# A four-stage fp32 chain on TensorE: three tile loads and one weight's sums moved in hand-written engine lists

## The chip, the cores and the metric

The kernel runs on one core of one Trainium2 chip. The metric is the device time of one execution in microseconds; the time before is the median of three.

## What is computed

Attention with a per-head decay (a retention layer) over 8 x 8 heads of 576 tokens and 64 dimensions, then two feed-forward blocks over the 4608 tokens:

```python
ret = scale * (q @ k.T) * Dmat          # Dmat = gamma ** (i - j) below the diagonal
x = (ret @ v) as [4608, 512]
h = max(max(x @ w1, x @ w2), x @ w3)    # w1..w3: 512 x 768
x = h @ w_out                           # 768 x 512
a, b = x @ u1, x @ u2                   # 512 x 1024
y = ((a * b) @ u3) @ u_out              # 1024 x 1024, 1024 x 512
```

The kernel multiplies u3 and u_out with each other first, beside the attention, so that the last two products are one of 1024 x 512.

## The kernel before, in words

After the attention four matrix stages follow, named B (the three products with w1 to w3 and their maximum), C (w_out), I (u1, u2 and their product) and O (u3 u_out). Each stage goes over six tiles of 768 tokens; a tile is read by 9, 2, 8 or 2 units (`PER_TILE`), each with a weight of its own. The units are numbered through: stage B has 0 to 53, C 54 to 65, I 66 to 113, O 114 to 125. Tiles are numbered through too (`tau`): 0 to 5, 6 to 11, 12 to 17, 18 to 23; so stage C's first tile is 6 and its third is 8, and weights 9 and 10 are stage C's, 11 to 18 stage I's, 19 and 20 stage O's.

A unit is a 2 x 2 block product done with seven products instead of eight (P1 to P7). So each tile is needed as seven blocks: four that are loaded (positions 0, 3, 6, 2, `load_raw`) and three sums of them, and a fourth sum that replaces position 3 (`combine`, four instructions on GpSimd that write positions 4, 1, 3, 5). Each weight is treated likewise: `load_weight` on SyncE (tiles `wraw` and `w21`), `sum_weight` (four instructions on GpSimd, counted by `w_summed`). fp32 accuracy comes from two rounded parts: ScalarE casts a block to its high part (`chi` for tokens, `whi` for weights), VectorE subtracts it from the block for the low part (`clo`, `wlo`), and TensorE multiplies high by high, high by low and low by high (lines 1261 to 1263).

The program has one loop over the iterations `it` = 0 to 126 on each engine, and within an iteration each engine's list is fixed; nothing is reordered at run time. TensorE does in iteration `it`: P1(it), P5(it-1), P4(it-1), P6(it), P3(it-1), P2(it), P7(it). ScalarE copies three partial results of a unit out of PSUM (`s`, `u`, `w`, lines 897, 918, 931), in places between them it casts blocks and weights; TensorE's P4 of a unit waits for that unit's copy `w`. VectorE adds PSUM to those copies (lines 1048, 1074, 1096) into `H`, which SyncE stores to HBM (`store`, line 623) for the next stage to load.

Where the side work stands is set by tables:

- `RAW_AT[it]`: in which iteration SyncE loads a tile. SyncE's list holds loads and stores, in one order.
- `T_AT[tau]`: in which iteration GpSimd does a tile's sums. In an iteration weights' sums come first, tiles' behind them.
- `W_LOAD_AT`, `W_SUM_AT`: a weight's load on SyncE, its sums on GpSimd.
- `W_HI`, `W_LO`: at which point of which iteration ScalarE casts the two parts of a weight, and VectorE subtracts them. Part 0 is what was loaded, part 1 the sums; the cast of part 1 waits for `w_summed`, and so does VectorE's subtraction of part 0.
- `due` and the tables above it: the same for the seven blocks of a tile.

Two lines set what a cast of a weight waits for, on ScalarE and on VectorE:

```python
                else:
                    act.wait_ge(w_summed, 4 * wi + 4)
...
                if part == 0:
                    dve.wait_ge(w_summed, 4 * wi + 4)
```

Stage I's blocks lie in memory over those of stage C (3072 bytes a block over 4608), so a load of stage I must wait until stage C's last tile was read there.

Of the kernel before, what the change touches and what calls it, by code (L numbers as in the profile page):

```python
# [25 lines left out]
TILES = TOKENS // (2 * N)  # L26
# [3 lines left out]
B, C, I, O = range(4)  # L30
# [46 lines left out]
def ends(g):  # L77
    return UNITS[g][2] % GROUP[stage(g)] == GROUP[stage(g)] - 1
# [37 lines left out]
def due(std, ci, io, it, point):  # L116
    out = []
    for tau in range(4 * TILES):
# [5 lines left out]
        if it == first_of(tau):  # L124
# [16 lines left out]
             18: 69, 19: 109, 20: 111}  # L141
W_SUM_AT = {2: 0, 3: 1, 4: 2, 5: 3, 6: 4, 7: 5, 8: 6, 9: 50, 10: 52, 11: 56, 12: 59, 13: 63, 14: 66, 15: 67, 16: 68,
            17: 69, 18: 70, 19: 110, 20: 112}
# [3 lines left out]
for _wi, _it in W_SUM_AT.items():  # L147
# [3 lines left out]
    else:  # L151
        _it += FIRST_W[I] <= _wi < FIRST_W[O]
        W_HI[_wi, 0], W_HI[_wi, 1] = (_it, "w"), (_it + 1, "s")
        W_LO[_wi, 0], W_LO[_wi, 1] = (_it + 1, "21"), (_it + 1, "21")
for _wi, _it, _later in ((9, 52, 0), (11, 56, 2), (12, 60, 2), (13, 64, 2)):
    W_HI[_wi, 0], W_HI[_wi, 1] = (_it, "p2"), (_it, "p2")
    W_LO[_wi, 0], W_LO[_wi, 1] = (_it, "12"), (_it + _later, "12")
# [10 lines left out]


RAW_AT = {}  # L170
T_AT = {}
for _tau in range(1, 4 * TILES):
    _st, _t = divmod(_tau, TILES)
    if _t == 0:
        _a = {C: 47, I: None, O: 107}[_st]
        T_AT[_tau] = {C: (50, 51), I: (65, 65), O: (109, 110)}[_st]
    elif _st in (B, I):
        _a = first_of(_tau - 1) + (4 if _tau == 1 else 2)
        T_AT[_tau] = (_a + 2, _a + 3)
    else:  # L180
        _a = first_of(_tau - 1)
        T_AT[_tau] = (_a, _a)
    if _a is not None:
        RAW_AT[_a] = _tau

# [81 lines left out]
def build(nc, qk, vv, vt, kk, wB, wC, wI, u3T, uo, decay, powers, columns, outT):  # L267
# [11 lines left out]
    with ctx:  # L279
# [132 lines left out]
        c_lo = sem("c_lo")  # L412
# [32 lines left out]
        def _(sp):  # L445
# [85 lines left out]
            def load_raw(tau, blocks=(0, 3, 6, 2)):  # L531
# [4 lines left out]
                else:  # L536
                    for i in range(2):
                        for j in range(2):
                            sp.wait_ge(stored[i][j], 16 * groups_through(tau - TILES))
                if t == 0:  # L540
                    sp.wait_ge(c_lo, 7 * tau)
                    if st == C:
                        sp.wait_ge(prod, DONE[(46, P3)])
                elif st in (B, I):
                    sp.wait_ge(c_lo, 7 * tau)
                else:
                    sp.wait_ge(combined, 4 * tau)
                for pos in blocks:
                    if t and st in (C, O):
                        if pos != 6 or st == O:  # L550
                            sp.wait_ge(c_lo, 7 * (tau - 1) + pos + 1)
                    load_raw_block(tau, pos)
# [72 lines left out]
            for it in range(G + 1):  # L625
# [9 lines left out]
                if g >= 0 and ends(g):  # L635
                    if begins(g):
# [4 lines left out]
                        if two_parts:  # L641
                            load_raw(tau, (0, 3, 6, 2) if tau // TILES == C else (0, 3, 2))
                        sp.wait_ge(sum12, g + 1)
                        store(g, 0, 1)
                    else:
# [4 lines left out]
                        if two_parts:  # L650
                            load_raw(tau, (0, 3, 6, 2) if tau // TILES == C else (0, 3, 2))
                        sp.wait_ge(merged12, ADDED[g])
                        store(g, 0, 1)
                if two_parts and tau // TILES == O:
                    load_raw(tau, (6,))
                if it < G and ends(it):
                    if begins(it):
                        sp.wait_ge(sum11, it + 1)
                    else:
                        sp.wait_ge(merged11, ADDED[it])  # L660
                    store(it, 0, 0)
                if it == 64:
                    load_raw(I * TILES)
                if tau is not None and not two_parts and not at_once:
# [7 lines left out]
        def _(pool):  # L672
# [24 lines left out]
            def combine(tau, i):  # L697
# [4 lines left out]
                if i == 0:  # L702
# [4 lines left out]
                    if tau == 1:  # L707
                        pool.wait_ge(w_lo, 2 * FIRST_W[C] - 1)
                    if again:
                        pool.wait_ge(c_lo, 7 * (tau - 1) + 5)  # L710
# [652 lines left out]
```

## Time and profile before

| | |
|---|---|
| time, median of 3 | 1230.83 us (1230.39 to 1232.71) |
| profiled execution | 1231.38 us, its span 1229.5 us |
| TensorE: matmuls, weight loads | 1222.1 us (99%), 1202.2 us (98%) |
| VectorE, ScalarE, GpSimd | 60%, 40%, 35% |
| HBM | 106.27 MB read, 61.87 MB written |

The profile counts a matmul as busy from issue to its modelled end, 335 ns, and they are issued twice as densely; so a gap of TensorE is best seen as idle time before a weight load (`PEld`). SyncE (`SP`) only issues transfers: its rows give when a transfer is issued, not when it lands. A time line row reads start, length, engine, line, operation, tiles, count, and in brackets how long the engine was idle before and what ended it.

### The profile page before, as it was taken

To read this page: it belongs to the slowest core of one execution; us is meant where nothing else is said; L and a number is where in the kernel's file an instruction comes from. 1 tells how busy PE (TensorE), PEld (TensorE's weight loads), DVE (VectorE), ACT (ScalarE), POOL (GpSimd) and SP (SyncE) were. 2 spreads that over 40 slices of the span, in tenths; PEclk is the share of its full clock that TensorE was granted. 3 is DMA by queue.
4 is the path that set the end of the run, shared out by engine and by line. 5 is a ranking of instruction groups with operands and counts; after the bars stand their busy time and mean duration, and the time that the engine had idled before them with its cause. 6 is when DMAs were issued, how large, how long until landed. Compare 5 with 4: busy or idle time off the path is not lost. (4 is left out here: it accounts for less than half of the span.)

```text
span 1229.5 us, 21665 instructions
## 1 busy us (share of the span) xinstructions
PE 1222.1 (99%) x8594; PEld 1202.2 (98%) x8594; DVE 737.7 (60%) x1065; ACT 485.7 (40%) x781; POOL 433.3 (35%) x234
## 2 busy tenths in 40 slices
PE   9999999999999999999999999999999999999999
PEld 8899999999999999999999999999999999999998
DVE  6444648845545464668886777454545466786653
ACT  3433544523232232326655544242323234554441
POOL 3535528220201102053867761202020217366550
PEclk9999999999999999999999999999999999999999
DMA  9999934121203021054464441313131342444441
GB/s 346 337 337 353 336 125 146 52 78 38 92 26 104 26 70 60 34 173 144 152 228 171 160 157 52 104 52 110 52 116 53 109 179 96 154 155 161 159 157 65
DMA packets 87332, 169.55 MB, mean 138 GB/s; under 512 B 9272, under 2 KB 58680, under 8 KB 87232
## 3 DMA queue, kind: packets, MB, share of 16 engines
q1 hardware_dynamic: 87232, 168.17, 39.1%
q8 instruction: 68, 1.11, 0.4%
q14 instruction: 32, 0.26, 0.1%
HBM read 106.27 MB, written 61.87 MB: 137 GB/s over the span
## 5 line engine op out<-in xcount | busy, mean ns | idle before, releaser
L1261 PE MATMUL ps<-chi,whi 128*128 128x384 f32 x2016 | 674.4, 335 | 1.9 <-ACT w L931 0.7
L1263 PE MATMUL ps<-chi,wlo 128*128 128x384 f32 x2016 | 673.5, 334 | 0.0
L1262 PE MATMUL ps<-clo,whi 128*128 128x384 f32 x2016 | 673.4, 334 | 0.0
L674 POOL TENSOR_TENSOR raw<-raw,raw 128x768 f32<-128x768 f32 (+3 forms) x102 | 268.1, 2650 | 582.8 <-DMA raw<-xd 203.5
L1261 PEld LDWEIGHTS ps<-chi,whi 128*128 128x128 f32 x2016 | 378.4, 188 | 4.5 <-ACT w L931 1.4
L1262 PEld LDWEIGHTS ps<-clo,whi 128*128 128x128 f32 x2016 | 378.4, 188 | 0.0
L1263 PEld LDWEIGHTS ps<-chi,wlo 128*128 128x128 f32 x2016 | 378.4, 188 | 0.0
L940 DVE TENSOR_TENSOR clo<-raw,chi 128x768 fp32r<-128x768 f32 (+2 forms) x168 | 253.5, 1537 | 41.7 <-ACT chi L851 41.7
L851 ACT CAST chi<-raw 128x768 fp32r<-128x768 f32 (+2 forms) x168 | 180.1, 1081 | 90.5 <-PE ps L1263 48.1
L931 ACT COPY w<-ps 128x384 f32<-128x384 f32 x126 | 60.5, 480 | 238.4 <-PE ps L1263 237.0
L918 ACT COPY u<-ps 128x384 f32<-128x384 f32 x126 | 60.7, 482 | 160.5 <-PE ps L1263 158.9
L1074 DVE TENSOR_TENSOR h<-ps,u 128x384 f32<-128x384 f32 x66 | 36.6, 555 | 122.8 <-PE ps L1263 121.2
L1048 DVE TENSOR_TENSOR h<-ps,w 128x384 f32<-128x384 f32 x66 | 36.6, 555 | 93.3 <-PE ps L1263 87.2
L1048 DVE TENSOR_TENSOR w<-ps,w 128x384 f32<-128x384 f32 x60 | 33.4, 557 | 87.0 <-PE ps L1263 86.9
L897 ACT COPY s<-ps 128x384 f32<-128x384 f32 x126 | 60.6, 481 | 55.5 <-PE ps L1263 55.5
L910 ACT COPY h<-ps 128x384 f32<-128x384 f32 x66 | 31.6, 479 | 82.4 <-PE ps L1263 79.8
L1074 DVE TENSOR_TENSOR u<-ps,u 128x384 f32<-128x384 f32 x60 | 33.3, 555 | 49.6 <-PE ps L1263 49.6
L674 POOL TENSOR_TENSOR wraw<-w,wraw 128x256 f32<-128x256 f32 (+2 forms) x21 | 26.2, 1247 | 95.2 <-DMA w<-wC 67.8
L940 DVE TENSOR_TENSOR wlo<-wraw,whi 128x768 fp32r<-128x768 f32 (+4 forms) x42 | 57.9, 1390 | 2.8 <-POOL wraw L674 2.7
L674 POOL TENSOR_TENSOR qdec<-qks,qtab 128x512 f32<-128x512 f32 x30 | 38.5, 1306 | 41.9 <-PE ps L1158 41.9
L952 DVE TENSOR_TENSOR probs<-ps,dec 128x512 f32<-128x512 f32 x64 | 39.9, 683 | 22.1 <-PE ps L1125 22.1
L674 POOL TENSOR_TENSOR wraw<-wraw 128x256 f32<-128x256 f32 (+2 forms) x42 | 47.4, 1129 | 1.6
(61 smaller groups left out, 820.7 us busy)
## 6 DMA issues: line engine op xcount, KB each, us to landing
gd<-h SPq DMA_DIRECT2D x96, 192.0 KB, 1.9
raw<-gd SPq DMA_DIRECT2D x24, 768.0 KB, 6.3
qks<-qk SPq DMA_DIRECT2D x30, 576.0 KB, 7.3
hd<-h SPq DMA_DIRECT2D x72, 192.0 KB, 1.9
raw<-hd SPq DMA_DIRECT2D x24, 576.0 KB, 6.6
x2d<-h SPq DMA_DIRECT2D x48, 192.0 KB, 2.9
raw<-x2d SPq DMA_DIRECT2D x24, 384.0 KB, 4.5
outT<-h SPq DMA_DIRECT2D x48, 192.0 KB, 1.9
```

Source lines behind the costliest of these rows:

```text
L674: return nc.gpsimd.tensor_tensor(out_, a, b, op)
L851: nc.scalar.copy(chi[st][pos][:, :, :], raw_block(tau, pos)[:, :, :]).then_inc(c_hi, 1)
L897: nc.scalar.copy(sbuf_s[it % 2][:, :], ps[:, X[it % 2], 0:N]).then_inc(s_made, 1)
L918: nc.scalar.copy(sbuf_u[it % 2][:, :], ps[:, X[it % 2], 0:N]).then_inc(u_made, 1)
L931: nc.scalar.copy(sbuf_w[it % 2][:, :], ps[:, X[it % 2], 0:N]).then_inc(w_made, 1)
L940: return nc.vector.tensor_tensor(out_, whole, hi.bitcast(f32), ALU.subtract)
L952: nc.vector.tensor_tensor(probs[n % 4][:, h, 0:NC * CH].rearrange("p (n c) -> p n c", c=CH), ps[:, 2 * (n % 2) + h, :].rearrange("p (n c) ...
L1048: nc.vector.tensor_tensor(to[:, :], ps[:, Z[g % 2], 0:N], sbuf_w[g % 2][:, :], ALU.add).then_inc(sum22, 1)
L1074: nc.vector.tensor_tensor(to[:, :], ps[:, Z[g % 2], 0:N], sbuf_u[g % 2][:, :], ALU.add).then_inc(sum12, 1)
L1261: nc.tensor.matmul(to, w1, x1, start=(start and k == 0), stop=False, skip_group_check=True)
L1262: nc.tensor.matmul(to, w1, x2, start=False, stop=False, skip_group_check=True)
L1263: last = nc.tensor.matmul(to, w2, x1, start=False, stop=(k == KH[st] - 1), skip_group_check=True)
```

## The change

Four moves, none of which adds or removes a computation:

1. Stage C's first tile (6) is loaded in iteration 48 instead of 47.
2. Weight 11's sums on GpSimd stand in iteration 57 instead of 56, and its casts and subtractions one iteration on as well.
3. Stage I's first tile (12) is loaded in iteration 64 behind the second store instead of behind all four, and each block waits only for the one block of stage C that lies last under it (`I_OVER`) instead of for all seven. GpSimd's first sum gets a wait of its own for the blocks under the one it writes.
4. Of stage O's second tile (19), block 0 is loaded in iteration 113, the rest in iteration 114 as before.

```diff
--- before.py
+++ after.py
@@ -139,7 +139,7 @@
           19: ((107, P3), 0), 20: ((110, P3), 18)}
 W_LOAD_AT = {2: 0, 3: 0, 4: 0, 5: 1, 6: 2, 7: 3, 8: 4, 9: 49, 10: 51, 11: 55, 12: 58, 13: 62, 14: 65, 15: 66, 16: 67, 17: 68,
              18: 69, 19: 109, 20: 111}
-W_SUM_AT = {2: 0, 3: 1, 4: 2, 5: 3, 6: 4, 7: 5, 8: 6, 9: 50, 10: 52, 11: 56, 12: 59, 13: 63, 14: 66, 15: 67, 16: 68,
+W_SUM_AT = {2: 0, 3: 1, 4: 2, 5: 3, 6: 4, 7: 5, 8: 6, 9: 50, 10: 52, 11: 57, 12: 59, 13: 63, 14: 66, 15: 67, 16: 68,
             17: 69, 18: 70, 19: 110, 20: 112}
 
 W_HI = {}
@@ -152,7 +152,7 @@
         _it += FIRST_W[I] <= _wi < FIRST_W[O]
         W_HI[_wi, 0], W_HI[_wi, 1] = (_it, "w"), (_it + 1, "s")
         W_LO[_wi, 0], W_LO[_wi, 1] = (_it + 1, "21"), (_it + 1, "21")
-for _wi, _it, _later in ((9, 52, 0), (11, 56, 2), (12, 60, 2), (13, 64, 2)):
+for _wi, _it, _later in ((9, 52, 0), (11, 57, 2), (12, 60, 2), (13, 64, 2)):
     W_HI[_wi, 0], W_HI[_wi, 1] = (_it, "p2"), (_it, "p2")
     W_LO[_wi, 0], W_LO[_wi, 1] = (_it, "12"), (_it + _later, "12")
 W_HI[2, 0] = (1, "s")
@@ -167,12 +167,15 @@
 
 
 
+I_OVER = {0: 0, 3: 2, 6: 4, 2: 1}
+
+
 RAW_AT = {}
 T_AT = {}
 for _tau in range(1, 4 * TILES):
     _st, _t = divmod(_tau, TILES)
     if _t == 0:
-        _a = {C: 47, I: None, O: 107}[_st]
+        _a = {C: 48, I: None, O: 107}[_st]
         T_AT[_tau] = {C: (50, 51), I: (65, 65), O: (109, 110)}[_st]
     elif _st in (B, I):
         _a = first_of(_tau - 1) + (4 if _tau == 1 else 2)
@@ -537,7 +540,9 @@
                     for i in range(2):
                         for j in range(2):
                             sp.wait_ge(stored[i][j], 16 * groups_through(tau - TILES))
-                if t == 0:
+                if t == 0 and st == I:
+                    sp.wait_ge(combined, 4 * tau)
+                elif t == 0:
                     sp.wait_ge(c_lo, 7 * tau)
                     if st == C:
                         sp.wait_ge(prod, DONE[(46, P3)])
@@ -546,6 +551,8 @@
                 else:
                     sp.wait_ge(combined, 4 * tau)
                 for pos in blocks:
+                    if t == 0 and st == I:
+                        sp.wait_ge(c_lo, 7 * (tau - 1) + I_OVER[pos] + 1)
                     if t and st in (C, O):
                         if pos != 6 or st == O:
                             sp.wait_ge(c_lo, 7 * (tau - 1) + pos + 1)
@@ -640,6 +647,8 @@
                         store(g, 1, 0)
                         if two_parts:
                             load_raw(tau, (0, 3, 6, 2) if tau // TILES == C else (0, 3, 2))
+                        if it == 64:
+                            load_raw(I * TILES)
                         sp.wait_ge(sum12, g + 1)
                         store(g, 0, 1)
                     else:
@@ -648,19 +657,19 @@
                         sp.wait_ge(acc21, ADDED[g])
                         store(g, 1, 0)
                         if two_parts:
-                            load_raw(tau, (0, 3, 6, 2) if tau // TILES == C else (0, 3, 2))
+                            load_raw(tau, (0, 3, 6, 2) if tau // TILES == C else (3, 2))
                         sp.wait_ge(merged12, ADDED[g])
                         store(g, 0, 1)
                 if two_parts and tau // TILES == O:
                     load_raw(tau, (6,))
+                if it == FIRST_UNIT[O] - 1:
+                    load_raw(O * TILES + 1, (0,))
                 if it < G and ends(it):
                     if begins(it):
                         sp.wait_ge(sum11, it + 1)
                     else:
                         sp.wait_ge(merged11, ADDED[it])
                     store(it, 0, 0)
-                if it == 64:
-                    load_raw(I * TILES)
                 if tau is not None and not two_parts and not at_once:
                     load_raw(tau)
             for i in range(2):
@@ -706,6 +715,8 @@
                         pool.wait_ge(x_out, 2 * PAIRS)
                     if tau == 1:
                         pool.wait_ge(w_lo, 2 * FIRST_W[C] - 1)
+                    if tau == I * TILES:
+                        pool.wait_ge(c_lo, 7 * (tau - 1) + 4)
                     if again:
                         pool.wait_ge(c_lo, 7 * (tau - 1) + 5)
                     if again == 1 and tau // TILES in (C, O):
```

ScalarE's list in iterations 56 and 57 (units' copies are `u`, `w`, `s`; `chi1_n` is position n of stage C's tile in turn, `whi11` weight 11). Before:

```order
L918 COPY u0_224<-ps 128x384 [waits sum12,prod]
L851 CAST chi1_6_84<-raw1_7_77 128x1152 [waits prod,raw_loaded2]
L834 CAST whi11_178<-wraw11_180 128x768 [waits w_loaded2]
L834 CAST whi11_178<-wraw11_180 128x1024 [waits w_summed]
L931 COPY w0_226<-ps 128x384 [waits sum22,prod]
L897 COPY s1_223<-ps 128x384 [waits sum11,prod]
L851 CAST chi1_0_78<-raw1_0_70 128x1152 [waits prod,raw_loaded0]
L910 COPY h10_220<-ps 128x384 [waits stored10,prod]
L918 COPY u1_225<-ps 128x384 [waits sum12,prod]
```

After:

```order
L929 COPY u1_225<-ps 128x384 [waits sum12,prod]
L862 CAST chi1_1_79<-raw1_1_71 128x1152 [waits prod,combined]
L862 CAST chi1_2_80<-raw1_2_72 128x1152 [waits prod,raw_loaded3]
L845 CAST whi11_178<-wraw11_180 128x768 [waits w_loaded2]
L845 CAST whi11_178<-wraw11_180 128x1024 [waits w_summed]
L942 COPY w1_227<-ps 128x384 [waits sum22,prod]
L862 CAST chi1_3_81<-raw1_3_73 128x1152 [waits prod,combined]
L908 COPY s0_222<-ps 128x384 [waits sum11,prod]
L862 CAST chi1_4_82<-raw1_4_74 128x1152 [waits prod,combined]
```

Both casts of weight 11 moved from ahead of unit 56's copy `w0` to ahead of unit 57's copy `w1`, behind the next tile's blocks 1 and 2.

GpSimd's list at the same place (`raw1_n` are the tile's blocks; tile 8 is the one that reads `raw1_6`). Before:

```order
L674 TENSOR_TENSOR raw1_5_75<-raw1_2_72,raw1_1_71 128x1152 [waits c_lo,combined,raw_loaded3]
L674 TENSOR_TENSOR wraw11_180<-w21_11_181,wraw11_180 128x256 [waits w_loaded2]
L674 TENSOR_TENSOR wraw11_180<-wraw11_180,w21_11_181 128x256
L674 TENSOR_TENSOR wraw11_180<-wraw11_180 128x256 [waits w_summed] x2
L674 TENSOR_TENSOR raw1_4_74<-raw1_3_73,raw1_0_70 128x1152 [waits c_lo,raw_loaded1,raw_loaded0]
L674 TENSOR_TENSOR raw1_1_71<-raw1_6_76,raw1_4_74 128x1152 [waits c_lo,combined,raw_loaded2]
L674 TENSOR_TENSOR raw1_3_73<-raw1_6_76,raw1_3_73 128x1152
L674 TENSOR_TENSOR raw1_5_75<-raw1_2_72,raw1_1_71 128x1152 [waits c_lo,combined,raw_loaded3]
```

After:

```order
L683 TENSOR_TENSOR raw1_5_75<-raw1_2_72,raw1_1_71 128x1152 [waits c_lo,combined,raw_loaded3]
L683 TENSOR_TENSOR raw1_4_74<-raw1_3_73,raw1_0_70 128x1152 [waits c_lo,raw_loaded1,raw_loaded0]
L683 TENSOR_TENSOR raw1_1_71<-raw1_6_76,raw1_4_74 128x1152 [waits c_lo,combined,raw_loaded2]
L683 TENSOR_TENSOR raw1_3_73<-raw1_6_76,raw1_3_73 128x1152
L683 TENSOR_TENSOR raw1_5_75<-raw1_2_72,raw1_1_71 128x1152 [waits c_lo,combined,raw_loaded3]
L683 TENSOR_TENSOR wraw11_180<-w21_11_181,wraw11_180 128x256 [waits w_loaded2]
L683 TENSOR_TENSOR wraw11_180<-wraw11_180,w21_11_181 128x256
L683 TENSOR_TENSOR wraw11_180<-wraw11_180 128x256 [waits w_summed] x2
```

Weight 11's sums moved from ahead of tile 8's four sums to behind them.

SyncE's list in iterations 46 to 50 (`hd<-h` are stores for stage C, `raw1` the loads of its first tile). Before:

```order
L623 DMA hd<-h01_219 128x384 [waits merged12]
L623 DMA hd<-h00_218 128x384 [waits merged11]
L528 DMA raw1_0_70<-hd 128x1152 [waits stored11,c_lo,stored10,prod,stored01,stored00]
L528 DMA raw1_3_73<-hd 128x1152
L528 DMA raw1_6_76<-hd 128x1152
L528 DMA raw1_2_72<-hd 128x1152
L623 DMA hd<-h11_221 128x384 [waits merged22]
L623 DMA hd<-h10_220 128x384 [waits acc21]
L623 DMA hd<-h01_219 128x384 [waits merged12]
L522 DMA wraw9_172<-wC 128x1152 [waits w_hi,w_summed,prod]
L523 DMA w21_9_173<-wC 128x384
L623 DMA hd<-h00_218 128x384 [waits merged11]
```

After:

```order
L630 DMA hd<-h01_219 128x384 [waits merged12]
L630 DMA hd<-h00_218 128x384 [waits merged11]
L630 DMA hd<-h11_221 128x384 [waits merged22]
L630 DMA hd<-h10_220 128x384 [waits acc21]
L630 DMA hd<-h01_219 128x384 [waits merged12]
L531 DMA raw1_0_70<-hd 128x1152 [waits stored11,c_lo,stored10,prod,stored01,stored00]
L531 DMA raw1_3_73<-hd 128x1152
L531 DMA raw1_6_76<-hd 128x1152
L531 DMA raw1_2_72<-hd 128x1152
L525 DMA wraw9_172<-wC 128x1152 [waits w_hi,w_summed,prod]
L526 DMA w21_9_173<-wC 128x384
L630 DMA hd<-h00_218 128x384 [waits merged11]
```

The four loads moved behind three stores, and stand now directly ahead of weight 9's load.

## Rows read from the trace of the kernel before

**Rows 1.** Page: granted clock of TensorE in 40 slices of the span

```profile
PEclk9999999999999999999999999999999999999999
```

**Rows 2.** Timeline of TensorE's weight loads: start, us, what, [idle before <-releaser]

```profile
532.01 0.19 PEld L1261 LDWEIGHTS ps<-chi,whi 128*128 128x128 f32 x1 [0.39 <-DVE h L1048]
...
599.64 0.19 PEld L1261 LDWEIGHTS ps<-chi,whi 128*128 128x128 f32 x1 [0.98 <-ACT w L931]
...
700.06 0.19 PEld L1261 LDWEIGHTS ps<-chi,whi 128*128 128x128 f32 x1 [0.95 <-ACT s L897]
...
704.04 0.19 PEld L1261 LDWEIGHTS ps<-chi,whi 128*128 128x128 f32 x1 [0.37 <-issue]
...
1065.17 0.19 PEld L1261 LDWEIGHTS ps<-chi,whi 128*128 128x128 f32 x1 [0.29 <-issue]
...
1077.97 0.19 PEld L1261 LDWEIGHTS ps<-chi,whi 128*128 128x128 f32 x1 [0.37 <-ACT w L931]
...
1084.85 0.19 PEld L1261 LDWEIGHTS ps<-chi,whi 128*128 128x128 f32 x1 [0.65 <-issue]
```

**Rows 3.** Timeline of SyncE from 519 us; landing times of the four block loads there

```profile
521.56 1.80 SPq L528 DMA_DIRECT2D raw<-hd  x4
...
527.35 0.50 SPq L522 DMA_DIRECT2D wraw<-wC  x1
...
DMA to landing us min/median/max: 3.6/5.8/7.8
```

**Rows 4.** Timeline of GpSimd, 535 to 556 us

```profile
535.44 1.02 POOL L674 TENSOR_TENSOR wraw<-w,wraw 128x384 f32<-128x384 f32 x1 [67.79 <-DMA w<-wC]
...
553.37 2.11 POOL L674 TENSOR_TENSOR wraw<-wraw 128x384 f32<-128x384 f32 x2
```

**Rows 5.** Timeline of VectorE and ScalarE, and of TensorE at 563.35 us

```profile
555.75 3.14 DVE L940 TENSOR_TENSOR wlo<-wraw,whi 128x1152 fp32r<-128x1152 f32 x2
...
559.11 1.49 ACT L834 CAST whi<-wraw 128x1536 fp32r<-128x1536 f32 x1
...
561.54 0.48 ACT L918 COPY u<-ps 128x384 f32<-128x384 f32 x1
...
563.35 0.33 PE L1261 MATMUL ps<-chi,whi 128*128 128x384 f32 x1
```

**Rows 6.** Timeline of GpSimd, 590 to 614 us

```profile
590.84 1.85 POOL L674 TENSOR_TENSOR wraw<-w,wraw 128x256 f32<-128x256 f32 x1
...
600.99 12.82 POOL L674 TENSOR_TENSOR raw<-raw,raw 128x1152 f32<-128x1152 f32 x4 [2.87 <-issue]
```

**Rows 7.** Timeline of ScalarE, 598 to 610 us, and of TensorE at 610.70 us

```profile
598.16 1.05 ACT L834 CAST whi<-wraw 128x1024 fp32r<-128x1024 f32 x1 [3.52 <-POOL wraw L674]
...
607.45 2.22 ACT L851 CAST chi<-raw 128x1152 fp32r<-128x1152 f32 x2 [3.87 <-POOL raw L674]
...
609.57 0.47 ACT L931 COPY w<-ps 128x384 f32<-128x384 f32 x1
...
610.70 0.33 PE L1261 MATMUL ps<-chi,whi 128*128 128x384 f32 x1
```

**Rows 8.** Timeline of GpSimd at 708 us: a weight's sum beside little VectorE work

```profile
708.72 0.73 POOL L674 TENSOR_TENSOR wraw<-wraw,w 128x256 f32<-128x256 f32 x1
```

**Rows 9.** Timeline of TensorE in the first 10 us

```profile
1.06 4.10 PE L1197 MATMUL ps<-idle 128*128 128x128 f32 x18 [1.06 <-DVE idle L1007]
...
8.20 1.05 PE L1197 MATMUL ps<-idle 128*128 128x128 f32 x8
```

**Rows 10.** Timeline of SyncE and of GpSimd before stage I

```profile
680.00 8.56 SPq L623 DMA_DIRECT2D x2d<-h  x3
...
693.12 8.57 POOL L674 TENSOR_TENSOR raw<-raw,raw 128x768 f32<-128x768 f32 x4 [7.46 <-DMA raw<-x2d]
```

**Rows 11.** Timeline of VectorE and of GpSimd around stage O's second tile

```profile
1040.12 2.56 DVE L940 TENSOR_TENSOR clo<-raw,chi 128x1536 fp32r<-128x1536 f32 x1
...
1066.27 16.85 POOL L674 TENSOR_TENSOR raw<-raw,raw 128x1536 f32<-128x1536 f32 x4 [18.56 <-DMA raw<-gd]
```

## The prediction

> **What bounds the kernel now.** I read the clock row first, then the waits of TensorE's weight loads, then the timelines of the other engines around each of those waits. The granted clock is full in all 40 slices [rows 1], so there is nothing to gain in rate. In the four stages TensorE runs its matmuls back to back, and the only time it loses stands in seven gaps before a weight load [rows 2]: 0.39, 0.98, 0.95, 0.37, 0.29, 0.37 and 0.65 us, together 4.0 us. The reader is to see that three of the parts of the change each sit beside one or two of these gaps, and that all of them together can give back no more than 4.0 us, 0.3% of the time. What a part can cost has no such limit: every engine works its list in order, and one wait put in the wrong place of ScalarE's list stops what TensorE needs from ScalarE behind it.
>
> All times below are in the clock of the profiled execution (1231.38 us, span 1229.5); the median of the three runs is 0.55 us lower, and I take that off at the end.
>
> **Part 1: stage C's first tile is loaded behind the stores.** Before, the four loads go out from 521.56 and the last lands 7.8 us after its issue, near 530.7 [rows 3]; three result stores wait in line behind them, VectorE cannot overwrite its buffer, and TensorE stands for 0.39 us at 532.01 [rows 2]. After, the stores go first, and that gap goes: -0.39. But the loads now start where weight 9's load did, at 527.35 [rows 3], 5.8 us later, and weight 9's load is queued behind them. Before, its data came at 535.44 [rows 4], 4.7 us behind the last block, of which some 1.5 us were the three stores, now gone. So it lands near 530.7 + 5.8 + 3.2 = 539.7, 4.2 us later. GpSimd is then busy without a pause until 555.48 (553.37 + 2.11, [rows 4]): weight 9's sums, the tile's four sums, weight 10's sums. Its end moves to 559.7, and further, because its last instructions now fall beside VectorE's two subtractions for weight 9, 3.14 us from 555.75 on [rows 5]; between "no overlap" (559.7) and "both subtractions in between" (562.8) I take 562. ScalarE's second cast of weight 10 waits for that end. It ran at 559.11 and the copy of u came at 561.54 to 562.02 [rows 5]; TensorE wanted that copy at 563.35 [rows 5]. ScalarE 2.9 us late, less 1.3 us of slack, but TensorE 0.4 us ahead: it stands 2.0 us. Net of the part: +1.6. Bounds: -0.4 (all hidden) and +2.8 (end at 562.8, and VectorE's backlog adds 0.4).
>
> **Part 2: weight 11's sums one iteration on.** Removed: ScalarE's second cast of weight 11 waits 3.52 us for GpSimd until 598.16, the copy of w comes behind it, and TensorE stands 0.98 us at 599.64 [rows 2, 7]. That gap goes: -0.98. Moved: the sums (four GpSimd instructions) now stand behind tile 8's four sums, and both casts of weight 11 stand one iteration on, ahead of that iteration's copy of w. Nothing lets tile 8's sums run sooner: they start at 600.99, when their blocks have landed (issued from 593.01, which itself waits for tile 7's sums, over at 590.84), and take 12.82 us, until 613.81 [rows 6]. GpSimd is in order, so weight 11's sums cannot begin before. ScalarE gets to the first cast behind the two token casts, at 609.67 (607.45 + 2.22, [rows 7]), does it in 0.8 us, and then waits. Before, the copy of w stood there at 609.57 and TensorE used it at 610.70 [rows 7].
>
> How long the wait is: beside VectorE's work one sum took 1.85 us [rows 6], four 7.3 us with the small waits between; with VectorE off the shared data it took 0.73 us [rows 8], four 3.0 us. Here VectorE is idle: its own subtraction for weight 11, put behind tile 8's second block, waits for the same sums, and all of its list stands behind that. So I take 3.0 us. For the same reason the last of tile 8's sums (3.2 us each on the mean of the 12.82) gets some 0.5 us shorter, so they are over at 613.3. The sums end at 616.3, the second cast (1.05) at 617.35, the copy of w at 617.8, and TensorE goes on at 617.8 instead of 610.70: +7.1, in which the -0.98 is already contained (the stall itself is 8.1 us). Other bound: sums at 1.85 each and no help for the tile's, 613.8 + 7.3 + 1.5 = 622.6, or +11.9. Lower bound: blocks of tile 8 landing 1 us sooner with everything uncontended, +5.5. The Trainium skill says in SBUF — State Buffer, section "Who interferes with whom", that VectorE and GpSimd share a port pair as an exclusive lock, and that whichever issues first holds it for its whole instruction. By that rule the four sums run alone here and the stall is the 8.1 us; by the nearest row in place (1.85 us each) it would be 12.9 us. The rows at 590.84 and 708.72 agree with the rule. The later casts are not a second stall: ScalarE is back 1.1 us behind TensorE after the copy of s and by the next copy of u has slack again.
>
> **The clock.** At 1.0 granted, the longest gap of these seven is 0.98 us; the new one is 8 us. The only row of a TensorE start after a long rest is the program's beginning: 18 equal matmuls took 4.10 us from 1.06 on, 0.228 us each, against 1.05 us for eight (0.131 each) from 8.20 on [rows 9]. At the later pace they would have taken 1.7 us less. The granted clock column prints full speed in that stretch, so that these ran at the lower level is read from the durations. I take +1.7 for the start after the 8 us stall; bounds 0 (clock kept) and +3.4 (twice that, since here the matmuls are back to back and longer). The Trainium skill, TensorE: Matmul & The Clock Gate, Part 1 says that an idle TensorE falls back to 1.2 GHz and that activity must win 2.4 GHz again. It speaks against this change; by it the price is paid, without it the sum is 1.7 us lower, and no stall in this trace is long enough to show it.
>
> **Part 3: stage I's first tile, block by block.** GpSimd waited 7.46 us for these blocks until 693.12; they were issued only behind the three stores that SyncE issued from 680.00 to 688.56 [rows 10]. Now they go behind the first of these, at 680 and, where a block waits for VectorE, up to about 684; GpSimd is free from weight 13's sums at 685.7 (693.12 - 7.46), and its tile sums run some 7 us sooner. The gaps of 0.95 and 0.37 us at 700.06 and 704.04 [rows 2] go: -1.3. GpSimd now works beside VectorE's subtraction for weight 13, whose sum follows for TensorE within half a us: +0.2 back. Net -1.1, bounds -1.3 and +0.5. The added wait on SyncE holds up one store by some 0.5 us, and its buffer is wanted 8 us later: nothing.
>
> **Part 4: stage O's second tile, one block sooner.** Block 0 needs tile 18's first block subtracted, which ends at 1042.68 [rows 11]; SyncE is free there, so it lands while nothing else is moved. GpSimd's wait until 1066.27 for blocks 0 and 3 [rows 11] then ends for block 3 alone, some 2.4 us sooner, and of the three gaps there (0.29, 0.37, 0.65) the last two hang on it and go: -1.0. The 0.29 us at 1065.17 hangs on weight 20's subtraction and stays. Bounds -1.0 and 0.
>
> **Sum.** +1.6 +7.1 +1.7 -1.1 -1.0 = +8.3 on 1231.38, which is 1239.7, or **1239.1 us** against the median of 1230.83: slower by 0.7%. 0.2% (2.5 us) is about what a measurement of this kernel can tell from no change.
>
> **Rivals.**
> 1. The stall without the rest: clock kept and part 1 hidden. 1230.83 - 0.4 + 7.1 - 2.1 = 1235.4. For it: the durations at the start are the only sign of the clock. Chance 0.22.
> 2. The stall with contended sums: +11.9 instead of +7.1, other terms as forecast, 1244.0. For it: the same sums took 7.3 us in place. Against: VectorE has nothing it may do. Chance 0.10.
> 3. Faster: ScalarE's wait for weight 11 is over before TensorE wants w. Then -0.4 - 1.0 - 1.3 - 1.0 = 1227.1. It decides at one point: tile 8's sums would have to end by 606 instead of 613.8 [rows 6], with their blocks landing 8 us sooner, though the issue waits for tile 7's sums at 590.84. Chance 0.05.
> 4. The change does not bring what it says: the stall is shortened by some loads landing early to about 3 us and the gains of 3.7 us cancel it, 1230. Chance 0.04.
>
> **How the numbers follow.** The forecast (stall of 7 to 9 us, most of the other terms) has 0.59. Slower by over 0.2%: forecast and rivals 1 and 2, 0.91; within: 0.04; faster: 0.05. The range goes from 1234.3 (rival 1 with the stall 1 us smaller) to 1244.5 (rival 2, or the forecast with both of the upper bounds of part 1 and the clock); rivals 3 and 4 and the ends beyond are the 2 in 10 left out.
>
> **What would show it.** In the profile after: one gap of TensorE of 7 to 9 us near 610 with ScalarE's copy of w as its releaser; ScalarE's cast of weight 11 waiting some 6 us for GpSimd's sum; those sums at 0.73 us each; matmuls at twice the spacing for a few us behind the gap, or not; GpSimd's first sum of weight 9 near 539.7 and a gap of 1 to 2 us near 563; no gaps near 532, 599.6, and at stage I's start. I am wrong if no gap of TensorE is over 3 us, or if tile 8's sums end well before weight 11's casts come up.

## The result, and the profile after

The change takes 1239.68 us (median of 6, 1238.96 to 1244.01) against 1231.25 us before (6 runs beside it): a ratio of 1.0077, with a 95% interval of 1.0058 to 1.0096. It is slower by 0.8%. One single run of those below, of the change without part 2, took 1332.49 us at a granted clock of 0.85 and is left out of every comparison. The profiled execution took 1238.96 us, its span 1237.0 us, 7.5 us more than the span before.

The page after, busy time of TensorE, VectorE and GpSimd and the granted clock, in 40 slices:

```profile
PE   9999999999999999999899999999999999999999
PEld 8899999999999999999799999999999999999998
DVE  6455648845455454658677768454545456776553
POOL 3535537220202011054666942202020216466550
PEclk9999999999999999999999999999999999999999
```

One slice of 40 has dropped on TensorE, the 20th, from 588 to 618 us. The clock row still prints 9 there; the stretches of 2 to 5 us further below show more. All gaps of TensorE's weight loads over 0.15 us in the four stages, from their timeline (columns as in [rows 2]):

```profile
560.91 0.19 PEld L1272 LDWEIGHTS ps<-chi,whi 128*128 128x128 f32 x1 [0.42 <-DVE w L1059]
564.25 0.19 PEld L1272 LDWEIGHTS ps<-chi,whi 128*128 128x128 f32 x1 [1.28 <-ACT u L929]
571.72 0.19 PEld L1272 LDWEIGHTS ps<-chi,whi 128*128 128x128 f32 x1 [0.21 <-issue]
573.92 0.19 PEld L1272 LDWEIGHTS ps<-chi,whi 128*128 128x128 f32 x1 [0.69 <-issue]
580.45 0.19 PEld L1272 LDWEIGHTS ps<-chi,whi 128*128 128x128 f32 x1 [0.31 <-issue]
617.80 0.29 PEld L1272 LDWEIGHTS ps<-chi,whi 128*128 128x128 f32 x1 [6.19 <-ACT w L942]
1073.63 0.19 PEld L1272 LDWEIGHTS ps<-chi,whi 128*128 128x128 f32 x1 [0.29 <-issue]
```

The gaps at 532, 599.6, 700, 704, 1078 and 1085 us [rows 2] are gone. Five small ones stand around the start of stage C (2.9 us together), and one of 6.19 us before unit 57's P4.

The timeline of GpSimd and then of ScalarE around that gap, which answers to [rows 6, 7]:

```profile
600.67 12.78 POOL L683 TENSOR_TENSOR raw<-raw,raw 128x1152 f32<-128x1152 f32 x4 [7.65 <-DMA raw<-hd]
613.40 0.72 POOL L683 TENSOR_TENSOR wraw<-w,wraw 128x256 f32<-128x256 f32 x1
614.08 0.72 POOL L683 TENSOR_TENSOR wraw<-wraw,w 128x256 f32<-128x256 f32 x1
614.76 1.53 POOL L683 TENSOR_TENSOR wraw<-wraw 128x256 f32<-128x256 f32 x2
...
609.25 0.83 ACT L845 CAST whi<-wraw 128x768 fp32r<-128x768 f32 x1
616.32 1.04 ACT L845 CAST whi<-wraw 128x1024 fp32r<-128x1024 f32 x1 [6.24 <-POOL wraw L683]
617.27 0.47 ACT L942 COPY w<-ps 128x384 f32<-128x384 f32 x1
```

ScalarE does the first cast, stands 6.24 us for weight 11's sums behind tile 8's, does the second, and only then copies w. The four sums took 0.72 us each.

TensorE in stretches (stretch, us, busy and count, granted clock, DMA share, GB/s):

```profile
610.00:615.00 5.00, 1.93 (x12) 1.00 0.00 0
615.00:620.00 5.00, 2.20 (x7) 0.68 0.22 73
620.00:622.00 2.00, 2.00 (x8) 0.50 0.83 273
622.00:624.00 2.00, 2.00 (x9) 0.59 0.25 89
624.00:626.00 2.00, 2.00 (x14) 1.00 0.91 242
```

The clock was at its lower level, 1.2 GHz (0.50), for 2 x 5 x 0.32 + 2.0 + 2 x 2 x 0.41 = 6.8 us, up to 623.6. TensorE worked from 617.80 on, so 5.8 us of matmuls ran at half speed and lost 2.9 us.

The balance, on the span: P4 of unit 57 starts at 617.80 instead of 610.70, +7.1; clock +2.9; gaps of stage I gone, -1.3; two of stage O's gone, -1.0; together +7.7 against 7.5 measured. This adds up, but it does not show that each term would come back if its cause were removed: for the clock and for the gaps of stages I and O the experiments say otherwise.

### The profile page after: what moved, and what is told of

The parts are those of the page before. It is cut to its first block, busy times and chain, and to the rows that moved or that the text cites. A ratio compares the mean times of both kernels' runs of the same rounds, so it can differ in the third digit from the quotient of the medians.

```text
span 1237.0 us, 21669 instructions
## 1 busy us (share of the span) xinstructions
PE 1224.9 (99%) x8594; PEld 1205.2 (97%) x8594; DVE 732.0 (59%) x1065; ACT 487.5 (39%) x781; POOL 429.3 (35%) x234
## 4 chain that ended last, share of the span: by engine, by line
PE 50%; POOL 1%; issue 0%; DVE 0%; ACT 0%; ACTq 0%; POOLq 0%
PE ps L1273 17%; PE ps L1272 17%; PE ps L1274 17%; POOL raw L683 1%; POOL wraw L683 0%; DVE h L1085 0%; ACT w L942 0%; ACTq L861 0%; POOLq L746 0%; ACT whi L845 0%; ACTq L905 0%
## 5 line engine op out<-in xcount | busy, mean ns | idle before, releaser
L951 DVE TENSOR_TENSOR clo<-raw,chi 128x768 fp32r<-128x768 f32 (+2 forms) x168 | 246.8, 1497 | 31.6 <-ACT chi L862 31.6
L951 DVE TENSOR_TENSOR wlo<-wraw,whi 128x768 fp32r<-128x768 f32 (+4 forms) x42 | 62.5, 1502 | 8.4 <-POOL wraw L683 8.3
L845 ACT CAST whi<-wraw 128x768 fp32r<-128x768 f32 (+4 forms) x42 | 43.8, 1052 | 11.5 <-POOL wraw L683 11.1
```

Of the source, the lines that this page charges most:

```text
L845: nc.scalar.copy(whi[wi][:, s, :, :], wraw[wi][:, s, :, :]).then_inc(w_hi, 1)
L951: return nc.vector.tensor_tensor(out_, whole, hi.bitcast(f32), ALU.subtract)
```

## The experiments

All ratios are against the kernel before, run beside it; each kernel has 5 to 12 runs. The kernels were compared on different chips, where the median of the kernel before was 1231.1 to 1231.7 us, so two kernels are best compared by their distance to it. The first group takes the change apart.

**Part 1 alone** (`C: 47` to `C: 48`).

> Part 1 alone (stage C's first tile loaded behind the stores). My theory: the 0.4 us gap near 532 goes, gaps of together 2.7 us come between 560 and 581 because weight 9's data lands 3 us later and its sums, the tile's and weight 10's follow; of these 2.3 us net the gap of 0.98 us near 599.6, which waits for GpSimd and not for TensorE, takes back up to 1: 1232 to 1233.5. Rival (the part only removes its gap): 1230.8. Rival (it carries the loss): 1239.

1233.44 us, ratio 1.0016 (1.0006 to 1.0027). The forecast for the part was +1.6; measured +2.0 (0.7 to 3.3). The gap at 532 is gone, and gaps of 1.10, 0.18, 0.69 and 0.32 us stand from 561 to 580. The three of 561 to 575 us (or a pair of 0.3 to 0.4 and 1.3 in place of the first) are in all profiles with this part and in none without it. One more came that nobody had asked for, 0.93 us at 604.89, with a subtraction on VectorE (weight 11's) that took 3.42 us at 600.50, where it took 0.94 before: GpSimd's sum had started at 599.80. Such a collision of VectorE's subtraction with GpSimd's sum returns below.

**Part 2 alone** (weight 11's sums and casts in iteration 57).

> Part 2 alone (weight 11's sums, casts and subtractions one iteration on, all else as before). My theory: this part is the whole loss. ScalarE waits in front of unit 57's copy of w for sums that stand behind tile 8's, TensorE goes on with unit 57's P4 near 617.8 instead of 610.7, one gap of some 8 us, then 5 to 7 us at half clock: 1231.2 + 7.1 + 2.9 = 1241.2 us (1240 to 1243). Rival (the loads of part 1 set the delay): at most 1 us slower than before.

1238.36 us, ratio 1.0058 (1.0041 to 1.0074). TensorE's gap is 6.19 us again, half clock for as long, but P4 of unit 57 starts at 616.40, 1.4 us sooner than forecast, and the time is below the 1240 to 1243 expected. The weight load at P4, and GpSimd's row for tile 8's first sum, which in the kernel before started at 600.99 [rows 6]:

```profile
616.40 0.29 PEld L1261 LDWEIGHTS ps<-chi,whi 128*128 128x128 f32 x1 [6.19 <-ACT w L931]
...
599.28 2.68 POOL L674 TENSOR_TENSOR raw<-raw,raw 128x1152 f32<-128x1152 f32 x1 [7.71 <-DMA raw<-hd]
```

SyncE issued the blocks at 593.71 here and at 593.01 before, and the first sum followed after 5.6 us instead of 8.0. It is tempting to put this down to weight 11's sums, which no longer run while the blocks are on their way. Part 1 alone speaks against that. It keeps weight 11's sums ahead of tile 8's, and there the first sum follows the issue (594.25) after 5.5 us as well:

```profile
594.25 2.21 SPq L528 DMA_DIRECT2D raw<-hd  x4
...
599.80 6.63 POOL L674 TENSOR_TENSOR raw<-raw,raw 128x1152 f32<-128x1152 f32 x2 [0.44 <-issue]
```

Over the profiles of all kernels this time lies between 5.4 and 8.0 us, and the kernel before has the longest. The prediction took that one value as fixed.

The gaps before stage I (700.06 and 704.04) and the one at 1077.97 are not in this profile either, though parts 3 and 4 are not in the kernel, and of the 0.65 us at 1084.85 only 0.16 are left. So in the change, where TensorE is late too, their absence does not show that parts 3 and 4 removed them.

**The change without part 2.**

> The change without part 2 (parts 1, 3 and 4). My theory: 1231.2 + 1.3 to 2.3 (part 1) - 1.3 (stage I) - 1.0 (stage O) = 1230.2 to 1231.2, the same as before within noise, and no stretch at half clock. Rival (part 1 or 3 is what costs): above 1236.

1232.51 us, ratio 1.001 (1.000 to 1.002), above the 1230.2 to 1231.2 expected. Its profile has no large gap and no half clock, only part 1's gaps, 0.99 us at 602.14 and two of 0.18 and 0.34 us: part 2 makes the stall, and the other three without it don't gain.

**TensorE kept at work during the stall.** 34 matmuls into an unused bank ahead of the wait for the copy of w; they add work that the result does not use.

```diff
+                    if g == 57:
+                        for _ in range(34):
+                            nc.tensor.matmul(ps[:, 4, 0:N], whi[10][:, 0, 0, :], whi[10][:, 0, :, :],
+                                             start=True, stop=True, skip_group_check=True)
                     pe.wait_ge(w_made, g + 1)
```

> The whole change, and TensorE does 34 further matmuls (into a PSUM bank that nothing reads) before its wait for unit 57's copy of w, 5.9 us of work in the 6.2 us gap. My theory: the gap's end is set by ScalarE and GpSimd, so P4 of unit 57 still starts near 617.8, but the clock stays full: 1239.7 - 2.8 = 1236.9, and the profile shows no half clock. Rival (the clock costs nothing, the slow matmuls overlap with other waits): 1239.7 as the change. Rival (the extra matmuls delay TensorE): over 1240.

1244.4 us, ratio 1.0105 (1.0085 to 1.0124): slower, where a gain was expected. The extra matmuls didn't delay TensorE: P4 came at 618.26, 0.31 us behind the end of its work and released by the copy of w. Behind it the clock stayed full:

```profile
610.00:615.00 5.00, 5.00 (x31) 5.00 (x30) 1.32 (x1) 0.46 (x1) 5.00 (x4) 1.00 0.00 0
615.00:620.00 5.00, 5.00 (x29) 4.69 (x29) 3.13 (x4) 3.22 (x5) 1.67 (x3) 1.00 0.15 50
620.00:625.00 5.00, 5.00 (x31) 5.00 (x30) 4.41 (x6) 3.67 (x5) 0.00 (x0) 1.00 0.65 180
```

(the five pairs are TensorE's matmuls and loads, VectorE, ScalarE, GpSimd). The copy of w one unit later starts at 626.37 instead of 628.57, although unit 57's P4 was 0.46 us later: at this point the full clock had brought 2.7 us. They were given back within 40 us, by gaps of 1.20 us at 644.38, 0.30 at 647.80 and 1.28 at 656.83 that the change doesn't have; the largest new gap then came in stage O. VectorE, GpSimd and TensorE there:

```profile
1071.78 5.58 DVE L951 TENSOR_TENSOR wlo<-wraw,whi 128x2048 fp32r<-128x2048 f32 x1
...
1071.10 4.10 POOL L683 TENSOR_TENSOR raw<-raw,raw 128x1536 f32<-128x1536 f32 x1 [14.39 <-DMA raw<-gd]
...
1077.47 0.29 PEld L1272 LDWEIGHTS ps<-chi,whi 128*128 128x128 f32 x1 [3.61 <-issue]
```

In the profile of the change the same two rows stand the other way round:

```profile
1071.23 2.28 DVE L951 TENSOR_TENSOR wlo<-wraw,whi 128x2048 fp32r<-128x2048 f32 x1
...
1071.60 5.27 POOL L683 TENSOR_TENSOR raw<-raw,raw 128x1536 f32<-128x1536 f32 x1 [15.43 <-DMA raw<-gd]
```

VectorE's subtraction for weight 20 takes 2.28 us when it is issued ahead of GpSimd's sum, by 0.37 us here, and 5.58 us when behind it, since it ends 2.2 us behind GpSimd's end (1075.20). VectorE's sums, which TensorE waits for, stand behind it in its list. The Trainium skill (SBUF — State Buffer, "Who interferes with whom") states that a VectorE instruction with two SBUF inputs contends with a GpSimd instruction that reads SBUF, that the port pair they share is an exclusive lock, and that the issue order decides who blocks; these rows agree.

The second group asks whether the harm of part 2 is the order on GpSimd or the place of the casts.

**Casts one iteration on, sums where they were** (after with `11: 56` in `W_SUM_AT`, `C: 47`).

> Weight 11's sums stay in iteration 56 ahead of tile 8's; only its two casts on ScalarE and its subtractions stand one iteration on, with parts 3 and 4 in and stage C's first tile loaded as before. Theory (the harm of part 2 is the order on GpSimd, not the place of the casts): the sums are over at 598 when ScalarE comes to the second cast at about 609, no wait is left on ScalarE, so the 0.98 us gap of before at 599.64 goes and no new one comes: 1231.2 - 1.0 - 1.3 - 1.0 = 1227.9 us, and at P4(57) no gap over 1 us. Rival (two casts, 1.85 us together, ahead of the copy of w already make TensorE wait, because only some 1.1 us lie between that copy and its use): a gap of about 0.7 to 1 us near 611, and 1228.8.

1233.96 us, ratio 1.0019 (1.0007 to 1.003). No gap over 1 us near 610, as the theory said, so the later casts alone don't make the stall; weight 11's sums have to stand behind tile 8's as well. But 0.40 us stay at P4 of unit 57, as in the rival, and gaps nobody forecast ate the rest (weight loads):

```profile
610.04 0.19 PEld L1272 LDWEIGHTS ps<-chi,whi 128*128 128x128 f32 x1 [0.40 <-ACT w L942]
613.87 0.19 PEld L1272 LDWEIGHTS ps<-chi,whi 128*128 128x128 f32 x1 [0.76 <-DVE h L1059]
637.64 0.19 PEld L1272 LDWEIGHTS ps<-chi,whi 128*128 128x128 f32 x1 [1.98 <-DVE h L1059]
641.07 0.19 PEld L1272 LDWEIGHTS ps<-chi,whi 128*128 128x128 f32 x1 [0.28 <-issue]
650.10 0.19 PEld L1272 LDWEIGHTS ps<-chi,whi 128*128 128x128 f32 x1 [1.24 <-DVE h L1059]
```

Ahead of the 0.76, 1.98 and 1.24 stands each time a subtraction of VectorE for a weight, 3.4 to 3.7 us long because it was issued behind a sum of GpSimd.

**Sums in 57, casts in 58** (after with `(11, 58, 2)`, `C: 47`).

> The change as it is, but weight 11's casts and subtractions one more iteration on (58), behind the sums instead of ahead of their end, and stage C's first tile loaded as before. Theory (the 8 us come only from ScalarE being made to stand still for sums that end at 616): ScalarE reaches the casts some 8 us later, about when the sums are over; no stall over 1 us, no half clock: 1228 us. Rival (weight 11's sums behind tile 8's hold GpSimd and VectorE up, so that the next tile's or weight 12's work comes late in any case): 1230 to 1232, with gaps in unit 58 or 59.

1231.65 us, ratio 1.0012 (0.9993 to 1.0031), single runs from 1228.85 to 1240.51. The stall near 610 is gone, as the theory said, though the sums still stand behind tile 8's. So it takes both: the sums late, and ScalarE made to stand for them ahead of a copy that TensorE needs. The profiled run, at 1240.51 the longest of the 12, has two other gaps, 2.48 us at 582.91 and 4.48 at 656.50, both behind subtractions held up by GpSimd (4.22 us at 578.58; two in 6.97 us from 648.54). The median lies in the rival's 1230 to 1232 us, but the gaps stand at the start of stage C and around unit 60, not in unit 58 or 59, and neither text foresaw the spread.

**Parts 3 and 4 alone.**

> The kernel before with parts 3 and 4 alone. The steps of the prediction: gaps at 700.06 and 704.04 go (-1.1 net), those at 1077.97 and 1084.85 go (-1.0): 1231.2 - 2.1 = 1229.1 us, and the gap at 599.64 stays at about 1 us. Rival (part 4 lets GpSimd's tile sums run into VectorE's subtraction for weight 20, as seen in the kernel with extra matmuls): some of the runs 3 to 5 us longer, about 1233 to 1234.

1231.03 us, ratio 0.9996 (0.9982 to 1.0009), from 1228.62 to 1235.43. The gaps at 700, 704, 1078 and 1085 are gone as forecast. The gain is not, in the median: the profile has a gap of 2.48 us at 581.51, at a place that neither part touches. (The gap at 599.64 is gone with it, against the expectation: TensorE comes there later than the copy of w.) VectorE and GpSimd:

```profile
577.18 4.22 DVE L951 TENSOR_TENSOR wlo<-wraw,whi 128x1536 fp32r<-128x1536 f32 x1
...
577.10 10.57 POOL L683 TENSOR_TENSOR raw<-raw,raw 128x1152 f32<-128x1152 f32 x3 [20.86 <-DMA raw<-hd]
```

Before, the same subtraction started at 576.41, 0.22 us ahead of GpSimd, and took 1.75 us. Here it was 0.08 us behind. Five profiled kernels do the same work up to this place: in three (before, part 2 alone, casts one iteration on) the subtraction came first, by 0.22 to 0.94 us, without a gap; in two (this one and the casts in 58) it came 0.08 and 0.10 us behind, with a gap of 2.48 us in both. So it is a race that the kernel before runs too.

The same gap can cost more than its length. TensorE's stretches (columns as above, the granted clock third from the end) with parts 3 and 4 alone, and then with the casts in 58:

```profile
580.00:585.00 5.00, 3.46 (x20) 3.49 (x21) 5.00 (x4) 1.52 (x2) 5.00 (x2) 1.00 0.35 119
585.00:590.00 5.00, 5.00 (x31) 5.00 (x30) 4.36 (x4) 3.20 (x5) 5.00 (x2) 1.00 0.42 150
...
580.00:585.00 5.00, 2.81 (x15) 2.52 (x14) 5.00 (x4) 0.48 (x2) 4.87 (x2) 0.94 0.41 147
585.00:590.00 5.00, 5.00 (x23) 5.00 (x23) 3.64 (x3) 2.00 (x3) 5.00 (x3) 0.72 0.71 216
```

The single runs agree. Of the 12 runs with parts 3 and 4 alone, the three above 1233 us, and only they, have a mean granted clock below 1.000 (0.998 and 0.999); of the 29 runs of the kernel before beside them it is the three longest (1234.10 to 1236.52 us).

**The change without part 4.**

> The change without part 4. By the prediction part 4 is worth -1.0, so 1239.7 + 1.0 = 1240.7 us. Second point: two of the six unprofiled runs of the change took 1244 us, the other four 1239 to 1240. If these come from stage O (GpSimd's sums of tile 19, started sooner by part 4, beside VectorE's subtraction for weight 20), no run here is at 1244 and all lie within 1240 to 1241.5. If they come from the stall in unit 57 or its clock, about a third of these runs are again 4 to 5 us above the rest.

1240.16 us, ratio 1.0069 (1.0053 to 1.0086), 1239.17 to 1242.34. That is 8.4 us above the kernel before beside it, as the change is above its own: nothing that a measurement can tell is left of part 4's 1.0 us. None of the six took 1244 us, but only two lie within the 1240 to 1241.5 expected.

The third group tests the race itself. GpSimd's first sum of tiles 7 and 19 already waits for VectorE's subtraction of the weight's first part; now for the second also:

```diff
-                        pool.wait_ge(w_lo, 2 * FIRST_W[tau // TILES] + 3)
+                        pool.wait_ge(w_lo, 2 * FIRST_W[tau // TILES] + 4)
```

**With parts 3 and 4:**

> Parts 3 and 4 alone, and GpSimd's first sum of the second tile of stages C and O (tiles 7 and 19) waits also for VectorE's subtraction of the second part of weight 10 or 20. In the profile with parts 3 and 4 alone that subtraction came 0.08 us behind GpSimd's sum (577.18 against 577.10), took 4.22 us instead of 1.75, and TensorE stood 2.5 us. Theory (whichever of the two issues first holds the other up): with the order fixed the subtraction takes 1.75 us in each run, the gap near 581.5 goes, GpSimd starts at most 1.75 us later, and the time is 1231.2 - 2.1 = 1229.1 us with a spread below 3 us. Rival (the 4.22 us come from something else that the order does not touch, or the later start of GpSimd gives the time back at the next tile): 1231 us as with parts 3 and 4 alone, with a gap of over 1 us between 575 and 610.

1230.11 us, ratio 0.9990 (0.9981 to 0.9999), 1229.03 to 1231.51: the spread is 2.5 us and the gap near 581.5 is gone, as the theory said; the size is 1 us short of it. That the wait narrows the spread isn't shown: with parts 3 and 4 alone it was 6.8 us, but the kernel before, which runs the race, spread over 7.3 us beside those runs and over 3.7 us beside these. The subtraction took 1.75 us at 576.14, and GpSimd started at 578.06 behind it. In this profile TensorE is not late before stages I and O, and of the gaps there only 0.19 us at 694.98 and 0.32 at 1063.94 are left: this is where parts 3 and 4 are seen to remove the gaps that they name. It is the lowest median of the study, 0.1% below the kernel before, less than what a measurement can tell here.

**With the filled stall:**

> The kernel with 34 extra matmuls ahead of the late copy, and with the same wait for tiles 7 and 19. Its profile without the wait had the subtraction for weight 20 at 5.58 us and TensorE standing 3.6 us and at half clock at 1077; the median was 1244.4. Theory: with the wait that subtraction takes some 2.3 us, that stall and its half clock (5.2 us together) go, and the time is 1239.2. Rival (the stall there has another cause): again 1244 us, with a gap of over 3 us near 1077.

1241.13 us, ratio 1.0086 (1.0072 to 1.01). The subtraction for weight 20 took 2.28 us at 1072.91, the gap near 1077 and its half clock are gone, and 3.3 us of 5.2 came back. Single runs still reached 1243.7 and 1245.0, with a granted clock of 0.999 and 0.998, so TensorE stood in these too; no profile shows where.

**With the change:**

> The change with the same wait for tiles 7 and 19. Theory (the two runs at 1244 us out of six are those in which GpSimd's sum of tile 19 comes ahead of VectorE's subtraction for weight 20): all runs within 1238 to 1241, median 1239.3. Rival (they come from the stall in unit 57 or from elsewhere): about a third again at 1243 to 1244.

1240.61 us, ratio 1.0075 (1.0063 to 1.0087), all five within 1240.07 to 1241.01: no run near 1244, but the median is 1 us above the change's. P4 of unit 57 comes at 619.03, after 7.28 us. Tile 8's blocks were issued only 0.24 us later than in the change (595.41), and the first sum followed after 6.8 us instead of 5.5. Beside this kernel the filled one with the same wait (1241.13) is no faster: the full clock behind the stall doesn't shorten the whole.

**A last one: parts 3 and 4, the wait, and weight 11's second cast alone behind the copy of w** (`W_HI[11, 1] = (56, "w")`).

> Parts 3 and 4 with the wait for tiles 7 and 19, and weight 11's second cast alone moved behind unit 56's copy of w instead of ahead of it; its sums stay in iteration 56, ahead of tile 8's, and VectorE's list is as before. Theory (the 0.98 us of before are ScalarE waiting for the sums with the copy of w behind that wait; moved like this, nothing that TensorE wants stands behind it, and no subtraction comes to lie beside other sums of GpSimd): the gap of 1.0 us at unit 56's P4 goes and none comes, 1230.1 - 1.0 = 1229.1 us. Rival (the cast now delays the copy of s by up to 1 us, or the time comes back as a shifted collision, as with the casts one iteration on): 1230 to 1231 us, with a gap of 0.5 us or more between 600 and 660.

1230.4 us, ratio 0.999 (0.998 to 1.000). The gap of 1.0 us at P4 of unit 56 went, and this came (a weight load, then VectorE and GpSimd):

```profile
604.12 0.19 PEld L1273 LDWEIGHTS ps<-chi,whi 128*128 128x128 f32 x1 [1.90 <-DVE h L1060]
...
599.68 3.46 DVE L952 TENSOR_TENSOR wlo<-wraw,whi 128x768 fp32r<-128x768 f32 x1
...
599.65 13.50 POOL L684 TENSOR_TENSOR raw<-raw,raw 128x1152 f32<-128x1152 f32 x4 [1.10 <-issue]
```

Weight 11's subtraction was 0.03 us behind GpSimd's sum. Before, it ran at 599.26, ahead of the sum at 600.99 [rows 6]. So in this profile the rival's shifted collision decided; single runs lie between 1228.28 and 1233.43 us.

## Why the prediction was right

The forecast was 1239.1 us for 1239.68, slower. By its steps:

- **Part 2, the mechanism and the place**: right. The gap stands at unit 57's P4 with the copy of w as releaser, the sums took 0.72 us each where 0.73 was taken, and they ended at 616.3. The rival with contended sums is out. P4 started at 617.80, the very number of the forecast.
- **That number is partly luck.** The step "Nothing lets tile 8's sums run sooner: they start at 600.99" failed: the first sum follows the issue after 5.6 us (part 2 alone) or 5.5 us (the change, from 595.17), not 8.0, and after 5.5 us too where weight 11's sums kept their place (part 1 alone). The 8.0 us of one profile were taken for a fixed time. The forecast also left out that part 1's delay moves that issue, from 593.01 to 595.17. The two cancel: 600.67 for 600.99. Part 2 alone shows the first error by itself: 616.40, not 617.8.
- **The stall's length**: 6.2 us, where 8.1 was said. Here an error of adding shows: part 1 had already made TensorE 2 us later when it came to the wait, and the end of the wait does not move with TensorE. The terms +1.6 and +7.1 share that time, since the +7.1 already ran to the absolute end at 617.8. Part 2 alone has a stall of 6.19 us too, with an end 1.4 us sooner; the blocks are issued 1.46 us sooner there, so what part 1 adds to the end of the stall is the later issue.
- **Part 1**: right in kind. Weight 9's sums started at 538.66 (539.7 said), weight 10's ended at 561.3 (562), and TensorE stood 1.28 us at 564.25, as "a gap of 1 to 2 us near 563". Not foreseen were 0.42 us before it and three gaps of 0.2 to 0.7 us behind it.
- **The clock**: right in kind, mis-sized. +1.7 was taken from the program's start; after this stall it was 2.9 us by the clock's stretches and 2.7 by the filled kernel, inside the bound of 3.4. Both are read close behind the stall; when the clock was kept there, the whole time did not get shorter. Rival 1 is out by its number: 1235.4 is below every run. Half of its mechanism came true, since part 1's cost did vanish in the stall.
- **Parts 3 and 4**: the named gaps went, -1.3 and -1.0, but most of that isn't theirs in this kernel: with part 2 alone the same gaps are gone but for 0.16 us, and without part 4 the change was no longer by what can be measured. By themselves the parts did not shorten the median by the 2.1 us forecast: 0.7 us against the kernel before beside them, 1.0 us with the order at tile 7 fixed, both less than a measurement can tell here. The race of VectorE with GpSimd at 577 us was not in the forecast at all.
- **The sum** came out near, +8.3 forecast and +7.7 by the balance, because a double count of 1.6 us stands against a clock term 1.2 us too small. That is luck.
- **The range**: its upper end of 1244.5 does not follow from "the forecast with both of the upper bounds of part 1 and the clock", which is 1239.1 + 1.2 + 1.7 = 1242.0; it rests on rival 2 alone.

**What stays open.** Two of the six runs of the change took 1244 us. No profile of such a run exists. Without part 4 (6 runs) and with the order fixed (5 runs) none of 11 did; that agrees with the race at 1071 us, whose other outcome the filled kernel shows, and doesn't prove it. What sets the 5.4 to 8.0 us between the issue of tile 8's blocks and the first sum, and with it the end of the stall, was not tested. Nor was why one gap of 2.48 us cost the clock and the other didn't.

## What to carry to other kernels

When an instruction is moved behind another engine's work, work out the time at which that work ends, not the length of a stall: delays ahead of the wait are swallowed by it, and they move the loads that the other engine waits for. For the same reason a gap that is gone in the profile of a change doesn't show that the part meant for it removed it; take the part alone. Before a long VectorE operation that TensorE depends on, look for what GpSimd starts within half a microsecond of it; if two rows are that close, the order is a race, one profile shows only one outcome, and a wait can fix the order. It holds GpSimd up for at most the subtraction's 1.75 us here, where the other order made TensorE stand 2.5 us. A stall of several microseconds on TensorE costs its clock as well.

## What the runs showed of the hardware

- After a stall of 6.2 us the granted clock was 0.50 for 6.8 us, of which 1 us lay still in the stall. With matmuls filling the same time it stayed at 1.00. A gap of 2.48 us at the start of stage C went with a full clock in one kernel and with 0.94 and 0.72 in the two stretches of 5 us from 580 us in another. In the filled kernel's stage O a gap of 3.61 us went with a granted clock of 0.65 and 0.67 in the two stretches of 5 us around it, 1075 to 1085 us.
- A subtraction of 768 elements on VectorE took 0.94 us ahead of GpSimd's sum and 3.46 us when issued 0.03 us behind it; 1536 elements 1.75 and 4.22 us (0.08 us behind). The loser waits for the whole sum of 2.7 us, so a shift of 0.3 us, from 0.22 ahead to 0.08 behind, decides over 2.5 us.
- The kernel before ran from 1229.2 to 1236.5 us in 29 runs of one comparison and from 1229.4 to 1233.1 in 17 of another. In both its longest runs, and only they, had a mean granted clock below 1.000: from 1234.10 us up in the first, the one at 1233.14 in the second.
